# Three changes to a one-core kernel of a Fourier mix and two feed-forward layers: 90 products of zeros at its head, a new split of the early copies, and a new order of its last products

## The chip, the cores and the metric

The kernel runs on one core of a Trainium2 chip. The metric is the device time of one execution in microseconds (us); the median of three runs of the kernel before is 1939.97 us. Engines are called PE (TensorE), ACT (ScalarE), DVE (VectorE), POOL (GpSimd) and SP (SyncE, which only issues transfers here).

## The reference

```
X = fft(fft(x, axis=1), axis=2).real          # x: 4 x 3008 x 256, float32
h = X.reshape(12032, 256) @ moe_w_in          # 256 x 2048
y = (relu(h) ** 2) @ moe_w_out                # 2048 x 256
h = y @ moe2_w_in                             # 256 x 2048
out = (h * cos(h)) @ moe2_w_out               # 2048 x 256, 12032 rows out
```

## The kernel before

The transform along the rows of the sequence is a product with cosine and sine tables (folded by symmetry, so that a batch needs tables of 378 columns for even and for odd frequencies). The transform along the 256 features is multiplied into the first weights once, at the start. Every float32 operand is split into a high and a low part (an ACT copy that rounds, then a DVE subtraction), and PE makes three products, high by high, high by low, low by high, of each pair (`three_passes`, L943; the products stand under L947).

After the start the work is a list of items (`schedule`, L109). There are 12 tiles of 502 columns. An **up** item of the first layer makes 128 hidden features of a tile (6 products), a **mix** item makes 256 of the second layer for one sign (12 products); each has a **down** step of 12 products that multiplies the activated values by the output weights. PE runs `up(it)` for an item and then `down` for the item two places back (`waiting`, L1123 to L1151), so that DVE and ACT have two items' time between the two. The instruction streams of the engines are written out by hand in program order and tied by semaphores; an instruction that waits holds everything behind it on its engine.

The parts around the change:

- The start of PE (L1013 to L1030): products of the first weights with the feature transform (`w1_product` L965 and L970, 12 products of 512 columns for each of four parts; `w128_product` L978, 4 products with 4 weight columns), then the first row transforms (`early_steps`, L998) from the even tables in the order 0, 1, 2 for the products of rows 0 and 1, and 3, 4, 5 for row 2, then the first up items.
- The six even tables (756 KB each) are loaded to `stage_t` and copied to `tab_even` as rounded numbers: tables 0, 2, 4, 5 by ACT (`table_parts`, L543 to L545), tables 1 and 3 by POOL (L935 to L939).
- The start of ACT (L567 to L600) makes the high parts in a fixed order: folded rows (`even_high`, L519), first weights (`w1_high`, L510), transformed weights (`weo_high`, L514), tables, row sums out of PSUM (`copy_odd_rows`, L536), the first tile's high part (L595). DVE has the low parts (L725, L731, L755), the folding (`fold_first`, L739 to L749), `take_rows` (L781 to L787) and the first tile's low part (L828).
- The odd tables (4536 KB) are copied from the input to a scratch in DRAM by one transfer from ACT's queue (`copy_odd_tables`, L547), issued ahead of the first item, loaded from there in two transfers at up item 6 (`load_odd_tables`, L554), and used by PE after the 16 up items of tile 0. The even tables are copied to the scratch in six transfers at up items 8 to 13 (`copy_even_tables`, L551), for later batches. Over SP's queue four small rows (`load_w128`, L385) come back as columns of `w128`, which DVE needs at up items 0, 4 and 6 (L893), and the output weights come in parts of 256 KB (`load_split`, L380), part n for ACT and DVE at up item n + 1 or n.
- At the end ACT makes the last high part (L619), DVE the last low part (L859), and PE runs the down steps of the last two items, each behind DVE's low part.

PE's order at its start is `w1_product(0)`, `w128_product(0)`, `w1_product(1)`, `w1_product(2)`; then for each of three tables the steps of row 0 and of row 1, then three steps of row 2 (each 6 products of 378 columns), then 8 products of `w128_product(1)` and `(2)`, two up items, `w1_product(3)` and `w128_product(3)`, and from there the items.

Of the kernel before, what the change touches and what calls it, by code (L numbers as in the profile page):

```python
# [11 lines left out]
ALU = mybir.AluOpType  # L12
ACT = mybir.ActivationFunctionType

P = 128
B, S, D, FF = 4, 3008, 256, 2048
# [3 lines left out]
KT = 3  # L20
KH = 378
KP = H // 2 + 1
T = 502
# [75 lines left out]

ODD_SUMS = {3: 0, 5: 1}  # L100

POOL_TABLES = (1, 3)

EVEN_COPIES = range(8, 8 + 2 * KT)

MADE_IN = {1: (1, 0), 2: (1, 1), 3: (2, 0), 4: (2, 1), 6: (3, 0), 7: (3, 1)}

# [26 lines left out]
def program(nc, ctx, x, x128, tables, consts, w1i, w1o, w2i, w2o, scratch_eo, scratch_a, scratch_t, out):  # L134
    def sem(name):
        return ctx.enter_context(nc.semaphore(name))
# [89 lines left out]
    weo_hi, weo_lo, row_done, row_out = sem("weo_hi"), sem("weo_lo"), sem("row_done"), sem("row_out")  # L226
    w128_in = [sem(f"w128_in{i}") for i in range(WQ)]

    c_hi, c_lo, te_hi, te_hi_pool = sem("c_hi"), sem("c_lo"), sem("te_hi"), sem("te_hi_pool")
    split_hi, split_lo = sem("split_hi"), sem("split_lo")  # L230
    tab_st, to_in = [sem("tab_st0"), sem("tab_st1")], [sem(f"to_in{i}") for i in range(2)]

# [6 lines left out]
    est0_st = sem("est0_st")  # L239
# [118 lines left out]
    def _(sp):  # L358
# [104 lines left out]
        store_rows(5)  # L463
        load_raw(1)
        sp.wait_ge(tab_st[0], 16 * 2 * KT)
        sp.wait_ge(tab_st[1], 16)
# [38 lines left out]
    def _(act):  # L505
# [10 lines left out]
        def even_high(kt):  # L516
            for phase in range(2):
                act.wait_ge(even0, 2 * kt + phase + 1)
                act.activation(f[phase][0][:, kt, :, 0, :], even_rows[phase][:, kt, :, :], ACT.Copy).then_inc(even_hi, 1)  # L519
# [27 lines left out]
        def copy_odd_tables():  # L547
            act.dma_start(scratch_t[1].rearrange("p t o h k -> (p t) (o h k)"),
                          tables[1].rearrange("p t o h k -> (p t) (o h k)")).then_inc(tab_st[1], 16)

        def copy_even_tables(n):  # L551
            act.dma_start(scratch_t[0, :, n], tables[0, :, n]).then_inc(tab_st[0], 16)

        def load_odd_tables():  # L554
            act.wait_ge(te_hi_pool, len(POOL_TABLES))
            act.wait_ge(tab_st[1], 16)
# [17 lines left out]
        even_high(0)  # L574
        w1_high(0)
        w1_high(1)
        even_high(1)
        w1_high(2)
        copy_w128(0)
        weo_high(0)  # L580
        table_parts(0)
        even_high(2)
        weo_high(1)
        table_parts(2)
        weo_high(2)
        copy_odd_rows(0)
        table_parts(4)
        copy_odd_rows(1)
        table_parts(5)
        w1_high(3)  # L590
        copy_odd_rows(2)
        act.wait_ge(odd0, 2)
        for phase in range(2):
            act.wait_ge(rows_out, phase + 2)
            act.activation(eo[0][:, phase, :], est0[:, phase, 0:T], ACT.Copy).then_inc(eo_hi, 1)  # L595
        copy_w128(1)
        split_high(0)

        act.wait_ge(a_in, 16)
        copy_odd_tables()  # L600

        half_pi = math.pi / 2

# [32 lines left out]
        def side_work(it):  # L636

            if row_taken(it) is not None:
                copy_odd_rows(row_taken(it))
            if fold_step(it) is not None:  # L640
                n, b, phase, piece, step = fold_step(it)
                if step == 3:
                    rows_high(n, piece // 2, piece % 2)
            for n in splits_in(it):
                if n == O2:
                    act.wait_ge(rows_done, number[0, 1, 1] + 1)
                elif n == O2 + 2:
# [4 lines left out]
            if it.t == 0 and it.kind == "up" and it.index == 6:  # L652
                load_odd_tables()
            if it.t == 0 and it.kind == "up" and it.index in EVEN_COPIES:
                copy_even_tables(EVEN_COPIES.index(it.index))

        pending = None
        for it in items:
# [63 lines left out]
    def _(dve):  # L722
# [52 lines left out]
        def take_rows(r):  # L775

            src, to, rows = row_sums(r)
            b, phase, odd = PRODUCTS[r]
            n, mirrored = columns_of(odd)
            dve.wait_ge(odd_copied, r + 1)  # L780
            dve.tensor_tensor(to[:, 0:n], src[0:rows, 0, 0:n], to[:, n:2 * n], ALU.add).then_inc(plus_done, 1)  # L781
            dve.wait_ge(plus_done, r + 1)
            even_part, odd_part = src[0:rows, 0, 0:mirrored], to[:, n:KP]
            if phase:
                dve.tensor_tensor(odd_part, odd_part, even_part, ALU.subtract).then_inc(rows_out, 1)  # L785
            else:
                dve.tensor_tensor(odd_part, even_part, odd_part, ALU.subtract).then_inc(rows_out, 1)  # L787

        def split_low(n):
            high, low = split_to(n)  # L790
# [19 lines left out]
        w1_low(0)  # L810
        w1_low(1)
        fold_first(1)
        even_low(1)
        w1_low(2)
        dve.wait_ge(wsp_lo, 3)
        weo_low(0)
        fold_first(2)
        even_low(2)
        weo_low(1)
        fold_odd()  # L820
        weo_low(2)
        take_rows(0)
        take_rows(1)
        w1_low(3)
        take_rows(2)
        for phase in range(2):
            dve.wait_ge(eo_hi, phase + 1)
            dve.tensor_tensor(eo[1][:, phase, :], est0[:, phase, 0:T], eo[0][:, phase, :].bitcast(F32),  # L828
                              ALU.subtract).then_inc(eo_lo, 1)

        def tile_low(t):
            dve.wait_ge(eo_hi, t + 2)
# [102 lines left out]
    @block.gpsimd  # L935
    def _(pool):
        for i, n in enumerate(POOL_TABLES):
            pool.wait_ge(t_in[n], 16)
            pool.tensor_copy(tab_even[:, n, :, :, :], stage_t[:, n, :, :, :]).then_inc(te_hi_pool, 1)  # L939

    @block.tensor
    def _(pe):
        def three_passes(out_, lhs, rhs, start, stop):  # L943
# [54 lines left out]
        def early_steps(r, kt):  # L998
            b, phase, odd = PRODUCTS[r]
            if odd:  # L1000
                pe.wait_ge(to_in[phase], 16)
            else:
                n = KT * phase + kt
                if n in POOL_TABLES:
                    pe.wait_ge(te_hi_pool, POOL_TABLES.index(n) + 1)
                else:
                    pe.wait_ge(te_hi, n + 1 - sum(m < n for m in POOL_TABLES))
            for parity in range(2):
                op = row_step(r, kt, parity, lambda i: tab[odd][:, KT * phase + kt, parity, i, :])
            if kt == KT - 1:  # L1010
                op.then_inc(rows_done, 1)

        w1_product(0)  # L1013
        w128_product(0)
        w1_product(1)
# [41 lines left out]

        def up(it):
            out_ = hb[it.c % 2]
            if it.c == 0:  # L1060
                pe.wait_ge(rows_out, EARLY)
            if it.kind == "up":
                for e in range(2):
                    if it.index == 0:
                        pe.wait_ge(eo_lo, it.t + 2 if it.t else e + 1)
# [13 lines left out]
            op.then_inc(h_done, 1)  # L1079

        def down(it):
            place = it.n % 2
# [21 lines left out]
            else:  # L1104
# [9 lines left out]
                for half in range(2):  # L1114
                    lhs = [[w[:, f2 * D + half * P:][:, 0:P] for w in wo2[it.index]] for f2 in range(2)]
                    op = three_passes(yb[1 - it.sign][:, half, 0:T], lhs,
                                      [[x_[:, place, f2, :] for x_ in gh] for f2 in range(2)],
                                      it.index == 0, it.last)
                    if half == 0 and it is steps[-1]:
                        op.then_inc(half_done, 1)  # L1120
            op.then_inc(g_used, 1)

        waiting = []  # L1123
        for it in items:
            if it == "flush":
                for old in waiting:
                    down(old)
                waiting = []
                continue
            if it.c >= 2:  # L1130
# [16 lines left out]
            if it.kind == "mix" and it.t == 0 and it.sign == 0 and it.index == 1:  # L1147
                for kt in range(KT):
                    early_steps(BESIDE, kt)
            if len(waiting) == 3:  # L1150
                down(waiting.pop(0))  # L1151
            if row_pieces(it) is not None:
                later_rows(*row_pieces(it))
# [40 lines left out]
```

## Time and profile before

| | us |
|---|---|
| median of 3 runs | 1939.97 (1939.87 to 1940.5) |
| the profiled execution | 1940.68 |
| its span in the trace | 1938.9 |
| PE busy | 1922.5 (99%) |
| DVE busy | 1433.4 (74%) |
| ACT busy | 1259.2 (65%) |
| POOL busy | 3.3 (0%) |

The span is the time from the first to the last instruction of the trace; the execution's own time is 1.8 us longer. Times in rows are in us from the start of the span unless they are marked ns. A product's recorded duration runs past the start of the next one, so the pace of products is read from start to start.

### The profile page before, as it was taken

The numbers are of one execution on the slowest core, as the hardware profiler recorded it, in microseconds if no ns is written. First come the engines' busy times: TensorE is split into PE (matmuls) and PEld (weight loads), VectorE is DVE, ScalarE is ACT, GpSimd is POOL, SyncE is SP. The second block draws the span as 40 slices with busy tenths as digits, with TensorE's granted clock in tenths as the row PEclk, the third lists the DMA queues.
The fourth block names the chain that finished last, engine by engine and source line by source line (L and its number), as shares of the span: only waits on it lengthen the run. The fifth ranks groups of instructions, "written<-read, shape, count | busy, mean of one in ns | idle before, by whom it ended". The sixth has DMA issues, their size and how long they took to land.

```text
span 1938.9 us, 21326 instructions
## 1 busy us (share of the span) xinstructions
PE 1922.5 (99%) x8452; PEld 1591.4 (82%) x8452; DVE 1433.4 (74%) x1661; ACT 1259.2 (65%) x1319; POOL 3.3 (0%) x6
## 2 busy tenths in 40 slices
PE   7999999999999999999999999999999999999999
PEld 5888888888888888888888888888888888888887
DVE  7978777876876877767787687677677777677665
ACT  6867656765765765676676576576566667567554
POOL 0000000000000000000000000000000000000000
PEclk9999999999999999999999999999999999999999
DMA  9821113013112211100111311200000000000000
GB/s 334 283 78 44 63 40 103 28 36 120 65 41 91 73 52 67 54 6 15 40 38 35 110 55 52 91 30 6 11 22 6 11 22 6 1 22 1 1 11 22
DMA packets 37203, 105.82 MB, mean 55 GB/s; under 512 B 4232, under 2 KB 14728, under 8 KB 36752
## 3 DMA queue, kind: packets, MB, share of 16 engines
q1 hardware_dynamic: 35840, 90.53, 13.8%
q10 hardware_dynamic: 1264, 13.94, 2.0%
q8 instruction: 66, 1.08, 0.2%
q14 instruction: 33, 0.27, 0.0%
HBM read 85.91 MB, written 27.82 MB: 59 GB/s over the span
## 4 chain that ended last, share of the span: by engine, by line
PE 97%; DMA 1%; DVE 1%; ACT 1%; SPq 0%; issue 0%; DVEq 0%; ACTq 0%
PE ps L947 97%; DMA w<-wrow 1%; DMA x<-x 0%; ACT tab_even L545 0%; PE ps L965 0%; DVE gh L859 0%; DVE pq L742 0%; ACT wsp L510 0%; ACT weo L514 0%; PE ps L970 0%; DVE uv L745 0%; DVE wsp_last L725 0%; DVE weo L731 0%; DVE u L923 0%; DVE u L906 0%; PE ps L978 0%
## 5 line engine op out<-in xcount | busy, mean ns | idle before, releaser
L947 PE MATMUL ps<-gh,wo 128*128 128x502 f32 x4608 | 1122.8, 393 | 2.0 <-DVE gh L859 1.9
L947 PEld LDWEIGHTS ps<-gh,wo 128*128 128x128 f32 x4608 | 871.5, 189 | 190.8 <-DVE gh L859 4.0
L947 PE MATMUL ps<-y,wi 128*128 128x502 f32 x2304 | 555.3, 390 | 0.0
L947 PEld LDWEIGHTS ps<-y,wi 128*128 128x128 f32 x2304 | 434.7, 189 | 87.7
L906 DVE TENSOR_TENSOR u<-kbuf,ps 128x1004 f32<-128x1004 int32 x192 | 230.6, 1201 | 347.1 <-ACT kbuf L706 346.9
L859 DVE TENSOR_TENSOR gh<-u,gh 128x1004 fp32r<-128x1004 f32 x384 | 460.0, 1198 | 3.2 <-ACT u L698 2.1
L706 ACT ACTIVATE kbuf<-ps 128x1004 int32<-128x1004 f32 x192 | 193.7, 1009 | 350.4 <-PE ps L947 349.4
L691 ACT ACTIVATE u<-u 128x1004 f32<-128x1004 f32 x192 | 200.9, 1046 | 167.1 <-DVE u L900 166.9
L947 PE MATMUL ps<-eo,weo 128*128 128x502 f32 x1152 | 292.5, 389 | 0.4 <-DVE eo L828 0.4
L947 PEld LDWEIGHTS ps<-eo,weo 128*128 128x128 f32 x1152 | 216.8, 188 | 46.2 <-DVE est L785 1.0
L718 ACT ACTIVATE u<-u 128x1004 f32<-128x1004 f32 x192 | 200.5, 1044 | 65.5 <-DVE u L906 65.5
L894 DVE SCALAR_TENSOR_TENSOR kbuf<-ab,w,ps 128x502 f32<-128x502 f32 x192 | 141.7, 738 | 122.5 <-PE ps L947 121.2
L923 DVE SCALAR_TENSOR_TENSOR u<-ps,u 128x1004 f32<-128x1004 f32 x192 | 231.0, 1203 | 1.1 <-ACT u L718 1.1
L697 ACT ACTIVATE gh<-u 128x1004 fp32r<-128x1004 f32 x192 | 200.3, 1043 | 16.5
L619 ACT ACTIVATE gh<-u 128x1004 fp32r<-128x1004 f32 x192 | 199.0, 1037 | 15.6 <-DVE u L923 15.6
L698 ACT ACTIVATE u<-u 128x1004 f32<-128x1004 f32 x192 | 197.2, 1027 | 0.0
L899 DVE TENSOR_TENSOR u<-kbuf,ps 128x502 f32<-128x502 f32 x192 | 130.2, 678 | 6.6
L900 DVE TENSOR_TENSOR u<-kbuf,ps 128x502 f32<-128x502 f32 x192 | 128.7, 670 | 0.0
L947 PE MATMUL ps<-ring,fa 128*128 128x378 f32 x216 | 41.5, 336 | 0.0
L947 PEld LDWEIGHTS ps<-ring,fa 128*128 128x128 f32 x216 | 38.1, 189 | 1.9
L864 DVE TENSOR_TENSOR y<-ps,y 128x1004 fp32r<-128x1004 f32 x24 | 28.8, 1201 | 5.6 <-ACT y L626 5.5
L626 ACT ACTIVATE y<-ps 128x1004 fp32r<-128x1004 f32 x24 | 24.2, 1007 | 8.0 <-PE ps L947 8.0
(85 smaller groups left out, 327.0 us busy)
## 6 DMA issues: line engine op xcount, KB each, us to landing
ring<-scratch_t SPq DMA_DIRECT2D x72, 378.0 KB, 3.9
xin<-x SPq DMA_DIRECT2D x36, 512.0 KB, 3.4
out<-osb SPq DMA_DIRECT2D x23, 502.0 KB, 3.4
raw<-scratch_eo SPq DMA_DIRECT2D x11, 502.0 KB, 5.1
scratch_eo<-est SPq DMA_DIRECT2D x14, 376.5 KB
stage_t<-tables SPq DMA_DIRECT2D x6, 756.0 KB, 16.1
scratch_t<-tables ACTq DMA_DIRECT2D x1, 4536.0 KB, 18.4
tab_odd<-scratch_t ACTq DMA_DIRECT2D x2, 2268.0 KB, 12.0
```

The lines of the kernel that those rows point to most:

```text
L619: act.activation(gh[0][:, place, :, :], u[:, place, :, :], ACT.Copy).then_inc(g_hi, 1)
L691: act.activation(u[:, place, :, :], u[:, place, :, :], ACT.Relu).then_inc(relued, 1)
L697: act.activation(gh[0][:, place, :, :], u[:, place, :, :], ACT.Square)
L698: act.activation(u[:, place, :, :], u[:, place, :, :], ACT.Square).then_inc(g_hi, 1)
L706: act.activation(kbuf[:, place, :, :].bitcast(I32), hb[it.c % 2][:, :, 0:T], ACT.Copy, bias=0.25).then_inc(copied, 1)
L718: act.activation(u[:, place, :, :], u[:, place, :, :], ACT.Sin, bias=half_pi, scale=-2 * math.pi).then_inc(cosined, 1)
L859: dve.tensor_tensor(gh[1][:, place, :, :], u[:, place, :, :], gh[0][:, place, :, :].bitcast(F32), ALU.subtract).then_inc(g_lo, 1)
L894: dve.scalar_tensor_tensor(out=k, in0=ab[:, :], scalar=w128[:, it.index:it.index + 1], in1=h[:, 0, 0:T], op0=ALU.mult, op1=ALU.add).then_i ...
L899: dve.tensor_tensor(u[:, place, 0, :], k, h[:, 1, 0:T], ALU.add)
L906: dve.tensor_tensor(u[:, place, :, :], kbuf[:, place, :, :].bitcast(I32), h[:, :, 0:T], ALU.subtract).then_inc(u_done, 1)
L923: dve.scalar_tensor_tensor(out=u[:, place, :, :], in0=h[:, :, 0:T], scalar=2 * math.pi, in1=u[:, place, :, :], op0=ALU.mult, op1=ALU.mult) ...
L947: op = pe.matmul(out_, a, b, start=start and i == 0, stop=stop and i == len(todo) - 1)
```

## The change

1. PE waits for the first of two zero fills and makes 90 products of 124 by 124 zeros into a PSUM tile (`WARM_UP`), ahead of `w1_product(0)`.
2. POOL does nothing any more. ACT copies even tables 0, 1, 2, 3 and 5, DVE copies table 4 (`VECTOR_TABLE`). The order of the early steps on ACT and DVE is new, and `take_rows` for rows 1 and 2 first subtracts only the columns of the first tile (`tile_rows`), the others later (`finish_rows`). The first up item begins with the products of the tile's high part, and waits for its low part only after two of them.
3. The odd tables are copied to the scratch in six transfers at up items 2 to 7 in place of one ahead of the items; they are loaded at item 9 in place of 6; the six copies of the even tables go out at items 10 to 15 in place of 8 to 13.
4. At the end PE makes the up products of the last item ahead of the down step that stood before them. The last down step (`last_down`) makes the products of the high part first, and waits for the low part behind them in each half.

```diff
+VECTOR_TABLE = 4
+ODD_COPIES, ODD_LOAD, EVEN_COPIES = range(2, 2 + 2 * KT), 9, range(10, 10 + 2 * KT)
+WARM_UP = 90
 # ACT, start
-        even_high(1)
+        weo_high(0)
         w1_high(2)
         copy_w128(0)
-        weo_high(0)
+        even_high(1)
+        weo_high(1)
         table_parts(0)
+        weo_high(2)
         even_high(2)
-        weo_high(1)
+        table_parts(1)
         table_parts(2)
-        weo_high(2)
+        table_parts(3)
         copy_odd_rows(0)
-        table_parts(4)
         copy_odd_rows(1)
         table_parts(5)
         w1_high(3)
         copy_odd_rows(2)
...
-            act.wait_ge(rows_out, phase + 2)
+            act.wait_ge(tile_rows, phase + 1)
...
-        act.wait_ge(a_in, 16)
-        copy_odd_tables()
 # ACT, with the up items of tile 0
+                if it.index in ODD_COPIES:
+                    copy_tables(1, it.index - ODD_COPIES.start)
+                elif it.index == ODD_LOAD:
+                    load_odd_tables()
+                elif it.index in EVEN_COPIES:
+                    copy_tables(0, it.index - EVEN_COPIES.start)
 # DVE
+            if r in (1, 2):
+                subtract_rows(r, 0, T - n).then_inc(tile_rows, 1)
             else:
+                subtract_rows(r, 0, mirrored).then_inc(rows_out, 1)
...
         fold_first(1)
+        w1_low(2)
         even_low(1)
-        w1_low(2)
+        fold_first(2)
         dve.wait_ge(wsp_lo, 3)
         weo_low(0)
-        fold_first(2)
+        weo_low(1)
         even_low(2)
-        weo_low(1)
         fold_odd()
         weo_low(2)
+        dve.wait_ge(t_in[VECTOR_TABLE], 16)
+        dve.tensor_copy(tab_even[:, VECTOR_TABLE, :, :, :], stage_t[:, VECTOR_TABLE, :, :, :]).then_inc(te_hi_dve, 1)
         take_rows(0)
         take_rows(1)
-        w1_low(3)
+        finish_rows(1)
         take_rows(2)
...
+        finish_rows(2)
+        w1_low(3)
 # POOL
-        for i, n in enumerate(POOL_TABLES):
-            pool.wait_ge(t_in[n], 16)
-            pool.tensor_copy(tab_even[:, n, :, :, :], stage_t[:, n, :, :, :]).then_inc(te_hi_pool, 1)
 # PE
+        pe.wait_ge(zeroed, 1)
+        zeros = lastc[0][:, 4 * KT * B:]
+        for _ in range(WARM_UP):
+            pe.matmul(ps[0][0:P - B, 0, 0:P - B], zeros, zeros, start=True, stop=True)
         w1_product(0)
...
+            if it.c < 2:
+                pe.wait_ge(rows_out, it.c + 2)
             if it.c == 0:
-                pe.wait_ge(rows_out, EARLY)
+                for e in range(2):
+                    pe.wait_ge(eo_hi, e + 1)
+                    for i, w in enumerate(weo):
+                        pe.matmul(out_[:, e, 0:T], w[:, e, 0:P], eo[0][:, e, :], start=i == 0, stop=False)
+                    pe.wait_ge(eo_lo, e + 1)
+                    op = pe.matmul(out_[:, e, 0:T], weo[0][:, e, 0:P], eo[1][:, e, :], start=False, stop=True)
...
+                for f2 in range(2):
+                    for w in weights[f2]:
+                        pe.matmul(out_, w, high[f2], start=False, stop=False)
+                pe.wait_ge(g_lo, it.n + 1)
+                for f2 in range(2):
+                    op = pe.matmul(out_, weights[f2][0], low[f2], start=False, stop=f2 == 1)
...
-            if len(waiting) == 3:
+            if len(waiting) >= 3 and it is not steps[-2]:
                 down(waiting.pop(0))
```

## Rows read from the trace of the kernel before

**Rows 1.** The page: its span, and the chain that ended last, by engine.
```profile
span 1938.9 us, 21326 instructions
...
PE 97%; DMA 1%; DVE 1%; ACT 1%; SPq 0%; issue 0%; DVEq 0%; ACTq 0%
```

**Rows 2.** Waits of PE from 0 to 80 us: total, times, longest.
```profile
PE ps L965 <- ACT wsp L510: 9.6, 1, 9.6
PE ps L947 <- ACT tab_even L545: 1.1, 2, 0.7
```

**Rows 3.** Timeline of PE, 0 to 62 us: start, us, instructions, idle before.
```profile
9.58 3.78 PE L965 MATMUL ps<-wsp,cs 128*128 128x512 f32 x8 [9.58 <-ACT wsp L510]
...
14.86 1.33 PE L978 MATMUL ps<-wsp,cs 128*4 128x512 f32 x4
16.03 2.00 PE L965 MATMUL ps<-wsp,cs 128*128 128x512 f32 x8
...
18.79 2.03 PE L965 MATMUL ps<-wsp,cs 128*128 128x512 f32 x8
...
26.57 1.31 PE L947 MATMUL ps<-tab_even,lastc 128*128 128x378 f32 x6 [0.67 <-ACT tab_even L545]
...
35.46 3.00 PE L947 MATMUL ps<-eo,weo 128*128 128x502 f32 x12 [0.39 <-DVE eo L828]
...
43.73 3.11 PE L947 MATMUL ps<-gh,wo 128*128 128x502 f32 x12
...
57.46 3.00 PE L947 MATMUL ps<-gh,wo 128*128 128x502 f32 x12 [0.73 <-DVE gh L859]
```

**Rows 4.** Timeline of PE's weight loads, 26 to 30 us.
```profile
26.57 1.00 PEld L947 LDWEIGHTS ps<-tab_even,lastc 128*128 128x128 f32 x6 [0.98 <-ACT tab_even L545]
27.56 1.05 PEld L947 LDWEIGHTS ps<-tab_even,fa 128*128 128x128 f32 x6
```

**Rows 5.** PE's weight loads by form: count, busy us, mean ns of one.
```profile
L947 PEld LDWEIGHTS ps<-ring,fa 128*128 128x128 f32 x216 | 38.1, 189 | 1.9
```

**Rows 6.** Timeline of DVE, 0 to 62 us.
```profile
0.83 0.30 DVE L796 MEMSET lastc<- 128x124 f32 x2 [0.83 <-PEq L1178]
...
12.20 1.23 DVE L742 TENSOR_TENSOR pq<-x 128x1024 f32<-128x1024 f32 x1 [0.24 <-DMA x<-x]
...
19.98 2.30 DVE L742 TENSOR_TENSOR pq<-x 128x1024 f32<-128x1024 f32 x1
...
54.25 0.74 DVE L894 SCALAR_TENSOR_TENSOR kbuf<-ab,w,ps 128x502 f32<-128x502 f32 x1 [0.93 <-DMA w<-wrow]
```

**Rows 7.** Timeline of POOL, 0 to 75 us.
```profile
19.76 1.45 POOL L939 CAST tab_even<-stage_t 128x1512 fp32r<-128x1512 f32 x1 [19.32 <-DMA stage_t<-tables]
23.46 1.66 POOL L939 CAST tab_even<-stage_t 128x1512 fp32r<-128x1512 f32 x1 [2.25 <-DMA stage_t<-tables]
```

**Rows 8.** Timeline of ACT, 16 to 30 us.
```profile
25.07 1.46 ACT L545 ACTIVATE tab_even<-stage_t 128x1512 fp32r<-128x1512 f32 x1
```

**Rows 9.** The page's transfers: engine, count, KB each, median us to landing.
```profile
scratch_t<-tables ACTq DMA_DIRECT2D x1, 4536.0 KB, 18.4
tab_odd<-scratch_t ACTq DMA_DIRECT2D x2, 2268.0 KB, 12.0
```

**Rows 10.** The same view of the transfers of 60 to 100 us.
```profile
stage_a<-w2i SPq DMA_DIRECT2D x8, 256.0 KB, 8.4
```

**Rows 11.** Timeline of ACT, 84 to 136 us.
```profile
93.43 1.05 ACT L691 ACTIVATE u<-u 128x1004 f32<-128x1004 f32 x1 [0.90 <-DVE u L900]
```

**Rows 12.** Timeline of all engines, 1914 to 1937 us.
```profile
1919.81 2.94 PE L947 MATMUL ps<-gh,wo 128*128 128x502 f32 x12
...
1922.58 2.88 PE L947 MATMUL ps<-y,wi 128*128 128x502 f32 x12
...
1928.91 3.02 PE L947 MATMUL ps<-gh,wo 128*128 128x502 f32 x12 [0.67 <-DVE gh L859]
...
1932.42 3.05 PE L947 MATMUL ps<-gh,wo 128*128 128x502 f32 x12 [0.49 <-DVE gh L859]
```

More of the change, by code:

```diff
@@ L100 @@
 ODD_SUMS = {3: 0, 5: 1}
-POOL_TABLES = (1, 3)
-EVEN_COPIES = range(8, 8 + 2 * KT)
+VECTOR_TABLE = 4
+ODD_COPIES, ODD_LOAD, EVEN_COPIES = range(2, 2 + 2 * KT), 9, range(10, 10 + 2 * KT)
+WARM_UP = 90
 MADE_IN = {1: (1, 0), 2: (1, 1), 3: (2, 0), 4: (2, 1), 6: (3, 0), 7: (3, 1)}
@@ L227, in program @@
     w128_in = [sem(f"w128_in{i}") for i in range(WQ)]
-    c_hi, c_lo, te_hi, te_hi_pool = sem("c_hi"), sem("c_lo"), sem("te_hi"), sem("te_hi_pool")
+    c_hi, c_lo, te_hi, te_hi_dve = sem("c_hi"), sem("c_lo"), sem("te_hi"), sem("te_hi_dve")
     split_hi, split_lo = sem("split_hi"), sem("split_lo")
@@ L238, in program @@
     odd0, odd_sum, odd_hi, odd_lo = sem("odd0"), sem("odd_sum"), sem("odd_hi"), sem("odd_lo")
-    est0_st = sem("est0_st")
+    est0_st, tile_rows = sem("est0_st"), sem("tile_rows")
     rows_done, odd_copied, plus_done, rows_out, est_st = (
@@ L465, in _ @@
         sp.wait_ge(tab_st[0], 16 * 2 * KT)
-        sp.wait_ge(tab_st[1], 16)
+        sp.wait_ge(tab_st[1], 16 * 2 * KT)
         for t in range(1, NT):
@@ L545, in table_parts, with copy_tables @@
             act.activation(tab_even[:, n, :, :, :], stage_t[:, n, :, :, :], ACT.Copy).then_inc(te_hi, 1)
[L547 to L552, printed above, removed]
+        def copy_tables(odd, n):
+            act.dma_start(scratch_t[odd, :, n], tables[odd, :, n]).then_inc(tab_st[odd], 16)
         def load_odd_tables():
-            act.wait_ge(te_hi_pool, len(POOL_TABLES))
-            act.wait_ge(tab_st[1], 16)
+            act.wait_ge(te_hi_dve, 1)
+            act.wait_ge(tab_st[1], 16 * 2 * KT)
             for phase in range(2):
@@ L651, in side_work @@
                 odd_high(odd_step(it))
[L652 to L655, printed above, removed]
+            if it.t == 0 and it.kind == "up":
+                if it.index in ODD_COPIES:
[4 more added lines that the diff above has]
+                    copy_tables(0, it.index - EVEN_COPIES.start)
         pending = None
@@ L782, in take_rows, with subtract_rows, finish_rows @@
             dve.wait_ge(plus_done, r + 1)
-            even_part, odd_part = src[0:rows, 0, 0:mirrored], to[:, n:KP]
-            if phase:
-                dve.tensor_tensor(odd_part, odd_part, even_part, ALU.subtract).then_inc(rows_out, 1)
-            else:
-                dve.tensor_tensor(odd_part, even_part, odd_part, ALU.subtract).then_inc(rows_out, 1)
+            if r in (1, 2):
+                subtract_rows(r, 0, T - n).then_inc(tile_rows, 1)
+            else:
+                subtract_rows(r, 0, mirrored).then_inc(rows_out, 1)
+        def subtract_rows(r, first, last):
+            src, to, rows = row_sums(r)
+            b, phase, odd = PRODUCTS[r]
+            n = columns_of(odd)[0]
+            even_part, odd_part = src[0:rows, 0, first:last], to[:, n + first:n + last]
+            parts = (odd_part, even_part) if phase else (even_part, odd_part)
+            return dve.tensor_tensor(odd_part, *parts, ALU.subtract)
+        def finish_rows(r):
+            n, mirrored = columns_of(PRODUCTS[r][2])
+            subtract_rows(r, T - n, mirrored).then_inc(rows_out, 1)
         def split_low(n):
@@ L1003, in early_steps @@
                 n = KT * phase + kt
-                if n in POOL_TABLES:
-                    pe.wait_ge(te_hi_pool, POOL_TABLES.index(n) + 1)
+                if n == VECTOR_TABLE:
+                    pe.wait_ge(te_hi_dve, 1)
                 else:
-                    pe.wait_ge(te_hi, n + 1 - sum(m < n for m in POOL_TABLES))
+                    pe.wait_ge(te_hi, n + 1 - (n > VECTOR_TABLE))
             for parity in range(2):
@@ L1059, in up @@
             out_ = hb[it.c % 2]
+            if it.c < 2:
+                pe.wait_ge(rows_out, it.c + 2)
             if it.c == 0:
-                pe.wait_ge(rows_out, EARLY)
-            if it.kind == "up":
+                for e in range(2):
[4 more added lines that the diff above has]
+                    op = pe.matmul(out_[:, e, 0:T], weo[0][:, e, 0:P], eo[1][:, e, :], start=False, stop=True)
+            elif it.kind == "up":
                 for e in range(2):
                     if it.index == 0:
-                        pe.wait_ge(eo_lo, it.t + 2 if it.t else e + 1)
+                        pe.wait_ge(eo_lo, it.t + 2)
                     at_ = slice(it.index * P, (it.index + 1) * P)
@@ L1079, in up, with last_down @@
             op.then_inc(h_done, 1)
+        def last_down():
+            it = steps[-1]
+            pe.wait_ge(g_hi, it.n + 1)
+            for half in range(2):
+                out_ = yb[1 - it.sign][:, half, 0:T]
+                weights = [[w[:, f2 * D + half * P:][:, 0:P] for w in wo2[it.index]] for f2 in range(2)]
+                high, low = ([x_[:, it.n % 2, f2, :] for f2 in range(2)] for x_ in gh)
+                for f2 in range(2):
[4 more added lines that the diff above has]
+                    op = pe.matmul(out_, weights[f2][0], low[f2], start=False, stop=f2 == 1)
+                if half == 0:
+                    op.then_inc(half_done, 1)
+            op.then_inc(g_used, 1)
         def down(it):
@@ L1118, in down @@
                                       it.index == 0, it.last)
-                    if half == 0 and it is steps[-1]:
-                        op.then_inc(half_done, 1)
             op.then_inc(g_used, 1)
@@ L1126, in _ @@
                 for old in waiting:
-                    down(old)
+                    if old is steps[-1]:
+                        last_down()
+                    else:
+                        down(old)
                 waiting = []
```

2 lines of the change are left out of this document (removed).

## The prediction

> **What bounds the kernel now.** I read the page first: of a span of 1938.9 us the chain that ended last lies 97% on PE [rows 1]. So only two things can make this kernel shorter: fewer or faster products, and less time in which PE has nothing to do. The waits of PE say where that time is. Before 80 us there is one long wait, 9.6 us for the first weights, and 1.1 us for table copies [rows 2]. PE's timeline gives the rest: 0.39 us before the first up item, 0.73 us at 57.46 [rows 3]. From there PE runs without a gap until the last two down steps, which wait 0.67 and 0.49 us [rows 12]. What the change can win lies in the first 57.46 us and in the last 20.
>
> The same timeline shows a second loss. The first 12 products of 512 columns start at 9.58 and the next group at 14.86, which is 5.28 us, or 0.44 us each. The 12 products of the next part but one, from 16.03 to 18.79, take 2.76 us, 0.23 us each [rows 3]. PE runs at 1.2 GHz when it begins after 9.58 us of rest, and at 2.4 GHz some 5.5 us later. That costs 5.28 - 2.76 = 2.5 us.
>
> **The tail (part 4 of the change).** Down steps and mix ups of 12 products take 2.77 us each when they follow one another (1919.81 to 1922.58) [rows 12]. Now the last up goes ahead of the down step at 1919.81. Five groups of 12 are left from there, in either order. Before, the last of them ended at 1932.42 + 3.05 = 1935.47. Without a wait it ends at 1919.81 + 5 x 2.76 + 0.17 (the recorded end stands 0.17 past the next start) = 1933.8. The gain is 1.7 us if no wait comes back. The last item's hidden values then come at 1922.6 in place of 1925.3. ACT's copy, DVE's subtraction, the sine, the product and the high part follow. In between ACT's high part of the item before must wait until the down step two places back has let the buffer go, at 1925.5, 0.7 us later than it could start otherwise. Worked through, DVE's low part for the last but one step ends near 1927.8 and PE wants it at 1928.1. The last high part ends near 1930.0 and its low part near 1931.2. PE wants them at 1930.8 and 1931.7, since four products of the high parts stand ahead. All fit, the tightest by 0.3 us. Bounds 1.2 (the two idles come partly back) and 1.8; I take **1.7**.
>
> **The early steps (part 2).** POOL's two casts take 1.45 and 1.66 us from 19.76 and 23.46 [rows 7]. DVE's sum of 1024 elements took 1.23 us at 12.20 and 2.30 us at 19.98, beside the first cast [rows 6]. So a cast stops DVE for about 1.07 us, and this happens twice on the way to the first tile. The Trainium skill says the same in GPSIMD Engine Reference, in its table of specifications: GpSimd shares its SBUF interfaces with VectorE when an instruction there has two SBUF inputs. The trace agrees (2.30 us against 1.23).
>
> In exchange ACT copies five tables, where it copied four, at 1.46 us [rows 8], and DVE one. DVE's copy of 1512 elements has no row; its nearest is the sum of 1024 in 1.23 us, which scales to 1.8 us; 0.9 us is the other end if one input goes twice as fast. I take 1.8.
>
> I follow PE with products of zeros that have ended by 9.6 us. Part 0 takes 12 x 0.23 = 2.8 us and its four small products 1.2: 13.5. Parts 1 and 2 end at 13.5 + 2 x 2.76 = 19.1. Table 0 can be had then. Table 1 is late: ACT makes the high part of part 2 (1.0), two folded rows (0.7), then the table (1.4), from 19.3: 22.4. PE wants it at 19.1 + 12 x 0.175 = 21.2 and waits 1.2 us. The remaining 42 products of the row steps take 42 x 0.175 = 7.4 us [rows 4], and 8 small ones 2.2: the first up item starts at 22.4 + 7.4 + 2.2 = 32.0, before at 35.46 [rows 3]: 3.4 us earlier. Tables arrive every 1.85 us (POOL's casts of tables 1 and 3 start 3.7 us apart), so table 5 comes at 27.2 and is copied at 28.7, which is just when PE wants it: this transfer is what limits any further gain here. Behind the two ups the activations of the first item (three ACT passes and a subtraction, 4.2 us) set the first down step, 43.73 before, 40.5 now: 3.2 us.
>
> **The odd tables (part 3).** The 4536 KB copy lands after 18.4 us [rows 9] and ahead of the small rows for item 4, for which DVE waits 0.93 us [rows 6]; PE's 0.73 us at 57.46 follows from this. In parts of 756 KB there is room between them. That gives up to 0.9 us more, so the start gives 3.2 to 4.1 us; DVE is nearly always busy there, so I take 3.6. What the move can cost: the odd load, 12.0 us for each half, now runs at items 9 to 12, beside weight parts that took 8.4 us [rows 10]. A part that is issued at item 9 has three items of 4.1 us, some 12 us, and can queue behind the one before. I expect one of them up to 1.7 us late at ACT. ACT has 0.90 us of rest in an item [rows 11] and DVE's low part comes after, so PE should not see it: 0, bounds 0 and 1. The six added issues stand on ACT's queue beside its work: 0. The tables have some 10 us before their first use.
>
> **The products of zeros (part 1).** They start at 1.1 us, behind the first fill [rows 6], and the time of 90 is the unknown that decides. No row has a product under 378 columns. The periods, 0.230 us at 512 columns and 0.175 at 378, are 0.41 ns a column and 0.02 us: 0.07 us for 124, and 0.12 at 1.2 GHz. At such a price 5.5 us at the low level hold 46 and the other 44 take 3.1 us: the end is at 9.7 and costs nothing. The other bound: when PE restarts, the first weight load and five more take 0.99 us, so the first alone is 0.99 - 5 x 0.175 = 0.11 us [rows 4]. If each load must end before its product begins, and none is hidden, a product costs 0.11 us and 0.22 at the low level: 25 and 65 of them, and the end is at 13.8. I take the first price, because it is what all rows of running products show: their loads are hidden wholly.
>
> The Trainium skill, TensorE: Matmul & The Clock Gate, section LDWEIGHTS, has columns over 1.2 as the time of a load in ns. For 124 columns that is an estimate of 103 ns, and its weight is on the second price; by it alone the sum would be some 4 us worse.
>
> **The sum.** 1940.68 (the profiled execution) - 1.7 - 3.6 = 1935.4. The median of the runs stands 0.7 under the profiled execution, so 1934.7. I put the forecast at **1935.0**, since the end of the zeros at 9.7 leaves no reserve.
>
> **The rivals.** (a) The weight load sets the price, 0.11 us. The first weights' products start at 13.8 in place of 9.7, and everything behind them on the start's chain moves with it: 3.6 - 4.1 + 1.7 = 1.2 us of gain, 1938.8; with a low level that ends earlier, 1938. For it: the restart's 0.11 us. Against: hidden loads.
> (b) Slower: the products of zeros hold PE far past the first weights. A load is recorded with 189 ns [rows 5]. If that whole time is spent for each product, because the stream of 124 columns is too short to cover it, 14 run at the low level in 5.5 us and 76 take 14.4: they end at 21. First products then start 11.3 us late: 1946. The turning point is an end at 15.0, a mean of 155 ns each, where the other gains (5.3) are used up; from 18.9 the kernel is slower by over 0.2%. Against it: products of 378 columns start 175 ns apart, so 189 ns is not a spacing.
> (c) The products of zeros do not raise the clock, or it falls before the weights: 2.5 us lost again, 1937.2. Nothing in the rows tells zeros from data. It can be that this part does not do what it says.
> (d) A wait inside the up items of tile 0 comes back, for a weight part behind the odd load or for the odd copies at item 9: 1 to 3 us, 1936 to 1938.
>
> **How the numbers follow.** Forecast 0.50, (a) 0.27, (b) 0.13, (c) 0.05, (d) 0.05. A change under 0.2% (3.9 us) is about what a measurement of this kernel can't tell from none. Faster by more, under 1936.1: the forecast's case alone, 0.50. Within: (a), (c), (d) and the mildest of (b): 0.36. Slower by more, over 1943.9: 0.14. The range goes from 1933.6 (4.1 at the start, 1.8 in the tail and 0.5 for scatter) to 1941.5, which takes in (a), (c), (d) and zeros up to 16.5 us, and leaves out most of (b) and a little below.
>
> **What would show it.** In PE's timeline: 90 products that start at 1.1 and end by 10; first weights' products at 0.23 us each from 9.6 on; the first up item near 32; a wait of about 1 us for table 1; no DVE sum of 1024 elements over 1.3 us; no DVE wait for the small rows; the stream without a gap from about 54; no idle in the last 20 us and a last product that ends 1.7 us nearer to its neighbours. Wrong would be: first weights' products that start after 12, or at 0.44 us each, or PE idle between 55 and 110.

## The result, and the profile after

The changed kernel takes 1946.89 us (median of 6 runs, 1945.93 to 1947.65), the kernel before 1940.59 in its 6 runs. The ratio is 1.0033, 95% interval 1.002 to 1.0046: 6.3 us slower, where I had forecast 5 us faster. The spans of the two profiled executions differ by nearly the same, 1945.0 against 1938.9.

The page of the changed kernel, span and engines, and the chain by engine and by line:

```profile
span 1945.0 us, 21513 instructions
...
PE 1939.3 (100%) x8542; PEld 1608.6 (83%) x8542; DVE 1431.7 (74%) x1664; ACT 1260.5 (65%) x1320; POOL 0.2 (0%) x4
...
PE 98%; DVE 1%; ACT 1%; DMA 1%; issue 0%; DVEq 0%; ACTq 0%
PE ps L959 96%; PE ps L1029 1%; DMA stage_a<-w2i 1%; PE ps L977 0%; DVE gh L877 0%; PE ps L982 0%; DVE kbuf L912 0%; DVE u L917 0%; ACT u L692 0%; ACT u L699 0%; PE ps L1115 0%; DVE u L918 0%; ACT gh L698 0%; ACT tab_even L548 0%; PE ps L990 0%
```

PE is more busy than before and the kernel is longer: L1029, the products of zeros, is now 1% of the chain. The waits of PE, 0 to 80 us (in total, times, longest), against [rows 2]:

```profile
PE ps L1029 <- DVE lastc L810: 1.0, 1, 1.0
PE ps L959 <- DVE gh L877: 0.5, 1, 0.5
PE ps L959 <- ACT tab_even L548: 0.4, 1, 0.4
PE ps L959 <- DVE weo L732: 0.3, 1, 0.3
```

The 9.6 us for the first weights are gone, and so are most other waits. The timeline of PE tells what stands in their place, to be held against [rows 3]:

```profile
1.04 18.86 PE L1029 MATMUL ps<-lastc 128*124 128x124 f32 x90 [1.04 <-DVE lastc L810]
19.70 3.73 PE L977 MATMUL ps<-wsp,cs 128*128 128x512 f32 x8
23.22 1.14 PE L982 MATMUL ps<-wsp,cs 128*128 128x512 f32 x4
24.21 1.26 PE L990 MATMUL ps<-wsp,cs 128*4 128x512 f32 x4
...
34.10 1.30 PE L959 MATMUL ps<-tab_even,lastc 128*128 128x378 f32 x6 [0.38 <-ACT tab_even L548]
...
43.77 0.63 PE L1083 MATMUL ps<-eo,weo 128*128 128x502 f32 x2
...
52.38 3.01 PE L959 MATMUL ps<-gh,wo 128*128 128x502 f32 x12 [0.45 <-DVE gh L877]
...
65.13 2.88 PE L959 MATMUL ps<-gh,wo 128*128 128x502 f32 x12
```

The 90 products run from 1.04 to 19.70: 18.66 us, 207 ns each, from the first to the last. The weights' products start at 19.70 in place of 9.58, 10.1 us later, although ACT had the first weights ready near 10. And they are slow again: 8 of them take 3.52 us (19.70 to 23.22), 0.44 us each. So the products of zeros put the start back by 10 us and did not raise the clock. (The column of the granted clock shows 1.00 over all of this stretch, as in the profile of before. The trace's first record of the clock begins only at 23.3 us, where the spacing turns to 0.25 us; ahead of that record the level is to be read from the spacing of products.)

ACT waits 13.44 us for PE in this stretch, with DVE behind it:

```profile
24.41 1.03 ACT L517 ACTIVATE weo<-ps 128x1024 fp32r<-128x1024 f32 x1 [13.44 <-PE ps L982]
```

The other parts show nearly as forecast. DVE has no sum of 1024 elements over 1.23 us, and its copy of table 4 took 0.94 us. There is one late weight part, 1.48 us at ACT, at item 12:

```profile
28.48 1.22 DVE L743 TENSOR_TENSOR pq<-x 128x1024 f32<-128x1024 f32 x1
...
36.94 0.94 DVE L837 CAST tab_even<-stage_t 128x1512 fp32r<-128x1512 f32 x1
```

```profile
96.86 0.64 ACT L564 ACTIVATE wi<-stage_a 128x512 fp32r<-128x512 f32 x1 [1.48 <-DMA stage_a<-w2i]
```

The tail has no idle time left, against [rows 12]:

```profile
1922.23 2.94 PE L959 MATMUL ps<-gh,wo 128*128 128x502 f32 x12
1925.01 5.61 PE L959 MATMUL ps<-y,wi 128*128 128x502 f32 x24
1930.45 8.39 PE L959 MATMUL ps<-gh,wo 128*128 128x502 f32 x36
1938.68 1.08 PE L1115 MATMUL ps<-gh,wo 128*128 128x502 f32 x4
1939.60 0.62 PE L1118 MATMUL ps<-gh,wo 128*128 128x502 f32 x2
1940.06 1.07 PE L1115 MATMUL ps<-gh,wo 128*128 128x502 f32 x4
1940.97 0.62 PE L1118 MATMUL ps<-gh,wo 128*128 128x502 f32 x2
```

The books: the fourth down step stood at 57.46 and stands at 65.13, 7.7 later. The late part takes PE 0.27 more near 102. The last two mix ups started at 1917.08 and 1922.58; the first of the pair now starts at 1925.01, 7.9 later, and the last product ends at 1941.59 against 1935.47, 6.1 later: the tail gave 1.8. And 6.1 is the difference of the spans.

### The profile page after: what moved, and what is told of

It is laid out like the page before. It is cut to its first block, busy times and chain, and to the rows that moved or that the text cites. A ratio compares the mean times of both kernels' runs of the same rounds, so it can differ in the third digit from the quotient of the medians.

```text
span 1945.0 us, 21513 instructions
## 1 busy us (share of the span) xinstructions
PE 1939.3 (100%) x8542; PEld 1608.6 (83%) x8542; DVE 1431.7 (74%) x1664; ACT 1260.5 (65%) x1320; POOL 0.2 (0%) x4
## 4 chain that ended last, share of the span: by engine, by line
PE 98%; DVE 1%; ACT 1%; DMA 1%; issue 0%; DVEq 0%; ACTq 0%
PE ps L959 96%; PE ps L1029 1%; DMA stage_a<-w2i 1%; PE ps L977 0%; DVE gh L877 0%; PE ps L982 0%; DVE kbuf L912 0%; DVE u L917 0%; ACT u L692 0%; ACT u L699 0%; PE ps L1115 0%; DVE u L918 0%; ACT gh L698 0%; ACT tab_even L548 0%; PE ps L990 0%
```

## The experiments

Theory 1 after this profile: the 90 products are the whole loss, they last twice what I took for them, and they leave the clock low because each spends its time on its load of 124 columns of weights and not on its stream of 124 columns. Its rivals: that the zeros, not the shape, leave the clock low; that small products have a floor of some 0.2 us; and that the new order loses time too. A further one is about the 207 ns itself: that a load of 124 columns takes 103 ns, one cycle a column at 1.2 GHz, and the stream of 124 columns another 103 ns behind it, with no overlap. It gives the same spacing as a load of two cycles a column that hides the stream.

Four kernels were run together, all from the changed one.

**No products of zeros.**

```diff
-WARM_UP = 90
+WARM_UP = 0
```

> The changed kernel with no products of zeros, all else as it is. Theory 1 (the 90 products take 18.9 us, from 1.0 to 19.9, and that is the whole loss): the first product of weights starts near 9.6 again, 10.3 us earlier, at 1.2 GHz for its first 5.5 us or so, which costs 2.5 us; the start then stands some 8 us below the changed kernel, so 1938.5 to 1939.5 here, and 1.5 to 2.5 us under the kernel before. Theory 2 (the new order of ACT and DVE or the moved tables lose time as well): over 1940.6. My forecast's own sum without the zeros: 1940.6 - 1.8 (tail) - 3.6 + 2.5 = 1937.7.

Measured: 1937.93 us, ratio to before 0.9984 (0.9975 to 0.9993), 2.7 us under the kernel before. So part 1 costs 9.0 us (6.3 and 2.7), more than the whole loss, and the other parts together gain 2.7. Theory 1 holds. Its number was a little high though the first weights came late in the profiled execution (PE started at 10.45); my forecast's own sum without the zeros, 1937.7, was nearer.

**40 products of zeros.**

```diff
-WARM_UP = 90
+WARM_UP = 40
```

> 40 products of zeros in place of 90. At 207 ns each they take 8.3 us and end at 9.4, just ahead of the first weights. Theory 1 (these products do not raise the clock): the first 12 products of weights take about 5 us again and the time is that of the kernel with none, within 0.5 us. Theory 1b (they raise it, only later than the 5.5 us seen, or the clock in the changed kernel rose late by chance): the first weights' products take 0.23 us each from about 9.6 on, and the time is 2 to 2.5 us below the kernel with none.

Measured: 1938.33 us, ratio 0.9987 (0.9978 to 0.9996), as with none. The timeline of PE:

```profile
1.04 8.53 PE L1029 MATMUL ps<-lastc 128*124 128x124 f32 x40 [1.04 <-DVE lastc L810]
9.91 3.72 PE L977 MATMUL ps<-wsp,cs 128*128 128x512 f32 x8 [0.34 <-ACT wsp L513]
13.46 1.09 PE L982 MATMUL ps<-wsp,cs 128*128 128x512 f32 x4
...
93.55 3.01 PE L959 MATMUL ps<-gh,wo 128*128 128x502 f32 x12 [0.90 <-DVE gh L877]
```

PE is now busy for 8.5 us ahead of the weights, and 8 products still take 3.55 us. Their count is right (they end in time) and the median gains nothing: the number 90 was not the only fault. The last line is a wait that the execution with no zeros does not have: PE stands 0.90 us behind the late weight part. So in this execution the late part took back most of the 1.2 us by which its fourth down step was earlier (55.36 against 56.53).

**19 wide products of zeros.** The same weights, the same 124 columns read four times.

```diff
-WARM_UP = 90
+WARM_UP = 19
+        wide = zeros.unsqueeze(1).broadcast_to([P, 4, P - B])
         for _ in range(WARM_UP):
-            pe.matmul(ps[0][0:P - B, 0, 0:P - B], zeros, zeros, start=True, stop=True)
+            pe.matmul(ps[0][0:P - B, 0, 0:4 * (P - B)], zeros, wide, start=True, stop=True)
```

> 19 products of zeros whose moving operand is the same 124 columns four times, 496 columns, in place of 90 of 124. At 1.2 GHz each takes 0.41 us, 7.9 us for 19. Theory A (small products spend half their time on the load of weights, and so little streaming does not raise the clock; zeros would): the clock rises during them or just behind, the first weights' products take 0.23 us each, 1.5 to 2.5 us below the kernel with none. Theory B (it is the zeros that do not raise the clock): the first 12 products of weights take about 5 us, as with none.

Measured: 1935.71 us, ratio 0.9973 (0.9963 to 0.9983), 4.9 us under the kernel before and 2.2 under the one with none. The timeline of PE:

```profile
1.04 7.01 PE L1030 MATMUL ps<-lastc 128*124 128x496 f32 x19 [1.04 <-DVE lastc L810]
9.86 2.13 PE L977 MATMUL ps<-wsp,cs 128*128 128x512 f32 x8 [1.81 <-ACT wsp L513]
11.83 1.08 PE L982 MATMUL ps<-wsp,cs 128*128 128x512 f32 x4
```

8 products of weights take 1.97 us, 0.25 each. The wide products themselves come 0.41 us apart up to 6.2 us and 0.22 apart from 6.5 on. Zeros raise the clock when they stream; theory A.

**40 products of a constant.** A tile of 124 columns filled with 1.37 ahead of the other fills.

```diff
...
+        dve.memset(filler[:, :].bitcast(F32), 1.37).then_inc(filled, 1)
...
-        pe.wait_ge(zeroed, 1)
-        zeros = lastc[0][:, 4 * KT * B:]
+        pe.wait_ge(filled, 1)
+        zeros = filler[:, :]
```

> 40 products of 124 by 124, as with 40 products of zeros, of a tile filled with 1.37. Theory A (shape): no difference from 40 of zeros, the clock stays low. Theory B (zeros): the clock rises within them, later ones come at about 104 ns in place of 207, they end before 8 us, and the first weights' products take 0.23 us each; 2 to 2.5 us below 40 of zeros.

Measured: 1938.81 us, ratio 0.999 (0.9981 to 0.9999). 40 take 8.53 us as with zeros, and 8 products of weights 3.58 (10.30 to 13.88). Zeros or 1.37 makes no difference here; both halves of theory A stand.

The second four took the parts one by one.

**The tail alone.** The kernel before with part 4.

```diff
+        def last_down():
...
-            if len(waiting) == 3:
+            if len(waiting) >= 3 and it is not steps[-2]:
```

> The kernel before with part 4 alone (last up ahead, last down step with its high products first). Theory 1 (the tail gains what the trace of the changed kernel shows, 1.8 us, and nothing else touches it): no idle in PE's last 20 us, 1.5 to 2 us below the kernel before. Theory 2 (the tail gives it back in the output): below 1 us.

Measured: 1938.38 us against 1940.28, ratio 0.9989 (0.998 to 0.9998): 1.9 us. PE has no wait after 80 us. Theory 1.

**The tables as before.** The changed kernel with no zeros, and part 3 undone.

```diff
-ODD_COPIES, ODD_LOAD, EVEN_COPIES = range(2, 2 + 2 * KT), 9, range(10, 10 + 2 * KT)
+ODD_COPIES, ODD_LOAD, EVEN_COPIES = (), 6, range(8, 8 + 2 * KT)
...
+        act.wait_ge(a_in, 16)
+        act.dma_start(scratch_t[1]..., tables[1]...).then_inc(tab_st[1], 16)
```

> The changed kernel without products of zeros and with the odd and even tables copied and loaded as before (one copy ahead of the items, load at item 6, even parts at 8 to 13). Against the changed kernel without zeros (1937.9) this is the worth of part 3. Theory 1 (the copy in parts takes away the wait for the small rows, 0.7 to 0.9 us of PE, and costs 0.27 us at the late weight part): 0.4 to 0.7 us slower, 1938.4, with PE idle once near 57 and not near 100. Theory 2 (DVE's chain sets the items' start anyway and part 3 gives nothing): the same within 0.3 us.

Measured: 1938.68 us, ratio 0.9992 (0.9983 to 1.0001), 1.6 under its kernel before where the one with part 3 was 2.7 under: by the medians part 3 is worth 1.1 us beside part 2. The two intervals overlap (the other is 0.9975 to 0.9993), so the medians alone do not show it. The traces do for the start: the fourth down step stands at 57.63, and at 56.53 with part 3. The timeline of PE, that of DVE, and the windows (behind the busy times of the five engines stands the granted clock):

```profile
57.63 4.55 PE L963 MATMUL ps<-gh,wo 128*128 128x502 f32 x12 [1.80 <-DVE gh L881]
```

```profile
54.43 0.74 DVE L916 SCALAR_TENSOR_TENSOR kbuf<-ab,w,ps 128x502 f32<-128x502 f32 x1 [2.00 <-DMA w<-wrow]
```

```profile
50.00:56.00 6.00, 5.83 (x26) 4.49 (x24) 3.97 (x6) 3.42 (x4) 0.00 (x0) 1.00 0.67 189
56.00:58.00 2.00, 0.37 (x2) 0.33 (x3) 2.00 (x3) 1.41 (x2) 0.00 (x0) 1.00 0.00 0
58.00:62.00 4.00, 4.00 (x12) 3.21 (x11) 3.96 (x7) 3.16 (x4) 0.00 (x0) 0.57 0.19 66
```

PE arrives earlier and the small rows do not: DVE waits 2.00 us for them, 0.93 before [rows 6]. PE's wait grows from 0.73 us [rows 3] to 1.80, and in this execution the granted clock fell behind it: 0.57 between 58 and 62, 12 products in 4.55 us in place of 3.0. This is the slowest of the 11 executions (1940.58 us) and the only one whose mean granted clock is not 1.0, so the fall is not in the median of 1938.68.

**Wide zeros on the kernel before.** 19 of them ahead of its `w1_product(0)`, nothing else.

```diff
...
+        for _ in range(19):
+            pe.matmul(ps[0][0:P - B, 0, 0:4 * (P - B)], zeros, wide, start=True, stop=True)
         w1_product(0)
```

> The kernel before with 19 wide products of zeros (496 columns) ahead and nothing else. The first 12 products of weights take 2.8 us in place of 5.3. Theory 1 (PE's start is bound by PE there): 2.2 to 2.5 us below the kernel before. Theory 2 (in the old order the folded rows of ACT and DVE and POOL's casts bound it): under 1.5 us, with longer waits of PE for tables and folded rows in its place.

Measured: 1939.87 us, ratio 0.9997 (0.9988 to 1.0006): 0.4 us, not to be told from none. The weights' first 12 products take 2.88 us (9.76 to 12.64). More than half of what was won is given back at the third table. The first table's products start 2.0 us earlier than before (19.57 against 21.59), those of the third 0.9 us (25.71 against 26.57), since PE waits 1.71 us there, against 0.67 in [rows 3]:

```profile
25.71 1.31 PE L947 MATMUL ps<-tab_even,lastc 128*128 128x378 f32 x6 [1.71 <-ACT tab_even L545]
```

and DVE's 512 elements beside POOL's cast took 1.82 us, where 0.69 is usual:

```profile
20.34 1.82 DVE L745 TENSOR_TENSOR uv<-pq 128x512 f32<-128x512 f32 x1
```

Theory 2: in the old order a clock that is up early is worth little. The profiled execution keeps 0.9 us of it (span 1938.0 against 1938.9), the median 0.4. In 5 of the 11 executions the mean granted clock is 0.999 in place of 1.0; none of these was profiled, so where it fell is not known.

**90 products with 4 columns of weights.** The changed kernel, its moving 124 columns as they are.

```diff
-            pe.matmul(ps[0][0:P - B, 0, 0:P - B], zeros, zeros, start=True, stop=True)
+            pe.matmul(ps[0][0:B, 0, 0:P - B], zeros[:, 0:B], zeros, start=True, stop=True)
```

> The changed kernel, its 90 products with 4 columns of weights in place of 124, the moving 124 columns as they are. Theory 1 (the load of 124 columns of weights sets the 207 ns, two cycles a column at 1.2 GHz): about 0.11 to 0.13 us each, the 90 end at 11 to 13 at the low level, and the kernel is 6 to 8 us faster than the changed one, 1939 to 1941. If the stream then fills enough of PE's time to raise the clock, they end near 8 to 9 and it is near 1936. Theory 2 (a product of this few columns has a floor of 207 ns whatever its weights): no change, 1946.9.

Measured: 1936.43 us, ratio 0.998 (0.9971 to 0.9989), 3.9 under the kernel before and some 10 under the changed one. The timeline of PE:

```profile
1.04 7.75 PE L1029 MATMUL ps<-lastc 128*4 128x124 f32 x90 [1.04 <-DVE lastc L810]
10.34 2.13 PE L977 MATMUL ps<-wsp,cs 128*128 128x512 f32 x8 [1.55 <-ACT wsp L513]
```

The same 90 products of 124 columns take 7.75 us and raise the clock: they come 103 ns apart up to 6.5 us and 56 ns apart from 6.6 on. This run leaves the stream as it is and takes 120 of the 124 columns of weights away (and with them all but 4 rows of the output, which no run takes apart from the load). So there is no floor of 0.2 us, it is the load that made 207 ns of each product, and with it the clock stayed low.

What the load costs alone can be estimated from the first product of a run, which nothing hides. With 124 columns of weights the second wide product starts 0.16 us later than the spacing of the others (0.575 us behind the first, 0.413 between the later ones); here the second starts 0.04 us earlier (0.063 and 0.103). The difference of 0.20 us for 120 columns is 1.7 ns a column, two cycles at 1.2 GHz. That speaks for the load of two cycles a column and against a load of one cycle with the stream behind it. It rests on recorded starts of one product in each run.

The last three ask for a better version, for the load's price at the high level, and for part 1 by itself.

**Wide zeros with the odd tables earlier.**

> The changed kernel with 24 wide products of zeros (they end near 9, so that PE rests less than 1 us before the weights) and with the odd copies at items 1 to 6 and the odd load at item 8 in place of 2 to 7 and 9. Theory 1 (the late weight part at item 12, 1.5 us at ACT, comes from the odd load beside it): no wait of ACT for a part over 0.5 us and PE's 0.3 us near 93 gone, 0.3 us below the kernel with 19 wide ones, 1935.4. Theory 2 (the late part only moves to item 11, where two parts are due): ACT waits there 1.5 us or more, and the time is equal or 0.5 us worse.

```diff
-ODD_COPIES, ODD_LOAD, EVEN_COPIES = range(2, 2 + 2 * KT), 9, range(10, 10 + 2 * KT)
+ODD_COPIES, ODD_LOAD, EVEN_COPIES = range(1, 1 + 2 * KT), 8, range(10, 10 + 2 * KT)
-WARM_UP = 90
+WARM_UP = 24
```

with the wide products as above. Measured: 1935.86 us, ratio 0.9977 (0.9968 to 0.9986), equal to the one with 19 (4.7 and 4.9 us under their kernels before). ACT still waits 1.5 us for one part and PE 0.2. The move of one item did not help; whether the odd load beside the parts causes the wait is not settled by it.

**16 wide and 15 narrow products.**

```diff
-WARM_UP = 90
+WARM_UP = 16
...
+        for _ in range(15):
+            pe.matmul(ps[0][0:P - B, 0, 0:P - B], zeros, zeros, start=True, stop=True)
```

> The changed kernel with 16 wide and then 15 of its own narrow products of zeros. The wide ones raise the clock near 6.5. Theory 1 (the load of 124 columns takes two cycles a column at either level): the narrow ones come 104 ns apart, 1.6 us for 15, and the first weights' products take 0.23 us each. Theory 2 (the load has a fixed time of about 0.2 us): 207 ns apart as in the changed kernel.

One execution of 1938.27 us. The timeline of PE and the windows:

```profile
1.04 5.42 PE L1030 MATMUL ps<-lastc 128*124 128x496 f32 x16 [1.04 <-DVE lastc L810]
6.30 1.74 PE L1032 MATMUL ps<-lastc 128*124 128x124 f32 x15
10.00 2.69 PE L977 MATMUL ps<-wsp,cs 128*128 128x512 f32 x8 [1.97 <-ACT wsp L513]
12.49 1.91 PE L982 MATMUL ps<-wsp,cs 128*128 128x512 f32 x4
```

```profile
9.00:12.00 3.00, 2.00 (x7) 1.65 (x8) 2.85 (x5) 1.90 (x3) 0.00 (x0) 0.89 1.03 410
12.00:14.00 2.00, 2.00 (x6) 1.46 (x5) 1.97 (x3) 0.00 (x0) 0.00 (x0) 0.50 1.03 422
```

The narrow ones come about 0.11 us apart at the high level, half of 207 ns: theory 1 for the price. Its second half fell: the clock was up, then fell to 0.50 again, after the narrow products and a rest of 1.97 us. With wide products alone a rest of 1.81 us did no such thing. One execution of each can't tell how much of it is the narrow products and how much chance. This time holds another loss: ACT waits 2.6 us for the late weight part, and PE 1.1 us behind it.

**90 products of zeros on the kernel before.**

```diff
...
+        for _ in range(90):
+            pe.matmul(ps[0][0:P - B, 0, 0:P - B], zeros, zeros, start=True, stop=True)
         w1_product(0)
```

> The kernel before with the 90 narrow products of zeros and nothing else. They end at 19.9 and put the first weights' products 10.3 us back. Theory 1 (the old order has 1.5 to 2.5 us of waits for tables and small rows that a late start hides): 7 to 9 us slower than before. Theory 2 (nothing is hidden): 10 us slower.

Measured: 1949.27 us against 1940.52, ratio 1.0044 (1.0028 to 1.0059), 8.7 us slower. PE's one long wait for a table is gone there (0.67 in [rows 3]), and the weights' first 12 products take 4.30 us in place of 5.28; the rest of the 10.1 us stays. The 4.30 is not a mark of the zeros: without any, these 12 took from 4.45 us (the tables as before) to 5.29 (the tail alone).

## Why the prediction was wrong

**The step that failed** is the price of a product of zeros. I put two prices side by side, 0.07 us (0.12 at the low level) from the stream and 0.11 us (0.22) from the load of weights, and took the first, "because it is what all rows of running products show: their loads are hidden wholly". Those rows have streams of 378 columns and more, 157 ns and up at the high level, over a load of 0.11 us. With 124 columns the stream is the shorter of the two and hides nothing of what the load takes beyond it. The row that bore on it was the restart [rows 4], and its price was right: 207 ns measured at the low level, 0.11 at the high one, and with the load taken away (4 columns of weights) the 90 end at 8.8. It was wrong to let the size of the group decide over the kind: the question was what comes out when the load is longer.

The Trainium skill's rule that I set beside it (TensorE: Matmul & The Clock Gate, LDWEIGHTS: columns over 1.2, 103 ns for 124) agrees with the 0.11 us at the high level. At the low level the measured 207 ns is twice that, which the rule does not say.

**The second fault** is a term that I carried over: "5.5 us at the low level". I gave rival (a) the load's price and (c) the clock that does not rise, and never the two together. The runs with wide products and with 4 columns of weights point to one cause for both: take the load's share away and the price falls and the clock rises. At the load's price and with no rise, 90 x 0.22 = 19.8 us, an end at 20.9: the measured end is 19.7. Rival (b) gave nearly this end (21) and this time (1946), on other grounds: it took the recorded 189 ns of a load for a spacing, and let the clock rise. The measured end lies past its turning point of 15.0 and past its 18.9, and the kernel is slower by 0.33%, where it says over 0.2%. No run ends near 15.0 itself. I gave it 0.13.

Rival (c) came true in what it says of the clock: in the changed kernel the products of zeros do not raise it. The reason that it hints at, zeros against data, is refuted: 19 wide products of zeros raise it, 40 narrow products of 1.37 do not.

**The rest of the sum came near, the start's term too high by 0.9 us.** With products that stream, the kernel is 4.9 us under its before by the medians, forecast 5.3 (1935.0 for the time, 1935.7 measured). The profiled execution is the slowest of its 8, and by spans the gain is 4.1 (1934.8 against 1938.9), as the trace's terms add up: 2.7 for the start, less 0.25 at the late weight part, and 1.8 for the tail. So that the median meets the forecast so well is in part luck. By terms:

- Tail: 1.7 forecast, 1.8 in the trace, 1.9 for the tail alone. The high products first and the buffer wait fell as worked out: ACT's high part waited 1.34 us for PE and no one saw it.
- First up item at 32.0: 32.55 with 19 wide products. The wait for table 1 was taken as 1.2 us in one place; it is 0.42 for table 0 and 0.36 for table 1. The fourth down step came 2.7 us earlier (54.78 against 57.46) and not 3.6, which is under my bounds of 3.2 to 4.1. The step that was short is the first down step, forecast 40.5 and measured 42.0; PE waits 0.59 us there for DVE.
- DVE's copy of 1512 elements took 0.94 us, at my lower bound, where I took 1.8; it lies beside other work.
- POOL's casts: no sum is stretched after they went.
- Part 3: 0.4 of my 3.6 us was its share. By the medians it is worth 1.1 us beside part 2, where the earlier start makes the wait for the small rows longer.
- The late part: 1.48 us at ACT (up to 1.7 forecast), 0.27 at PE (0 taken, bounds 0 and 1). PE's wait behind it differs from execution to execution: 0.90 us with 40 products of zeros, 1.17 with 40 of 1.37, 1.13 with wide and narrow ones, 0.17 with the odd tables earlier, and about 0.25 with 19 wide ones. It comes with part 3: the execution with the tables as before has no such wait. Rival (d) names it, at 1 to 3 us.

The gains are not a sum of parts: wide zeros alone give 0.4 us, parts 2 and 4 without them 1.6, of which the tail is 1.9, and all together 4.9. I read this so, that each of the start's parts alone only moves the wait to the next; single terms of 0.4 and 1.1 us are within what the intervals leave open.

## What to carry to other kernels

In these runs a product took the longer of its stream and its load of weights, so a group of small square products is a group of loads. To fill time ahead of the real work, stream wide: repeat the same columns, or take few columns of weights. Then look at what the next products cost, since being busy alone did not raise the clock; and count the filler by its price at the low level, because what runs past the first weights is lost nearly whole: a start 10.1 us later cost 9.0 us here and 8.7 in the old order.

## What the runs showed of the hardware

- Products of 124 columns with 124 columns of weights in this 4-byte type came 207 ns apart at 1.2 GHz and about 108 at 2.4 GHz. With 4 columns of weights they came 103 and 56 ns apart, 7.75 us for 90. As an estimate from these rows a load takes two cycles a column.
- PE was busy without a gap for 18.7 us with such products and stayed at 1.2 GHz (0.44 us for a product of 512 columns behind them). With products of 496 columns the spacing turned from 0.41 to 0.22 us within 19 of them, 7.0 us in all; these were zeros, and no wide products of other data were run.
- Once, behind a wait of 1.80 us in the middle of the stream, the granted clock was 0.57 over the next 4 us; once it fell to 0.50 some 1.3 us after a rest of 1.97 us. Rests of 1.81, 1.61 and 1.55 us ahead of the weights were not followed by a fall in their profiled executions. What decides it is open.
